# Leaving out the filler products on the tensor engine at both ends of an attention, MLP and soft-mixture kernel

## The reference, cut to what matters

```
# 1. chunked attention, B=4, H=8, S=768, D=64; chunks of 32 queries,
#    keys: 8 memory rows + 16 before the chunk + the chunk + 8 after it
a = softmax(q_c @ k_full.T / 8);  out[:, :, chunk] = a @ v_full
x = out as 3072 tokens x 512
# 2. MLP, 512 -> 2048 -> 512
h = x @ w_in;  g = h * sigmoid(h);  x = g @ w_out
# 3. soft mixture, 8 experts x 4 slots, 512 -> 1024 -> 512
logits = x @ phi                          # 3072 x 32
slot_input = softmax(logits, over tokens).T @ x
slot_out[e] = relu(slot_input[e] @ w1[e]) @ w2[e]
out = softmax(logits, over slots) @ slot_out
```

## Time and profile before

| | |
|---|---|
| median of 3 runs | 479.77 us (477.81 to 480.75) |
| the profiled execution's own time | 477.67 us |
| its span | 475.9 us |
| PE busy | 451.3 us, 95% of the span, 5460 passes |
| PE weight loads busy | 332.9 us, 70% |
| DVE, ACT, POOL busy | 275.0, 138.6, 45.3 us |
| DMA | 81.59 MB; share of the 16 engines 44.4% on average |
| chain that ended last | PE 85%, DMA 6%, DVE 4%, others 1% or less each |

### The profile page before, as it was taken

How to read it: one execution, slowest core, us unless ns; L and a number is a source line. 1 busy time by engine, 2 the same in 40 slices (tenths; PEclk the granted TensorE clock), 3 DMA queues, 4 the chain that set the end, 5 groups by cost and what they waited for, 6 DMA issues and landing times.

```text
span 475.9 us, 12278 instructions
## 1 busy us (share of the span) xinstructions
PE 451.3 (95%) x5460; PEld 332.9 (70%) x5460; DVE 275.0 (58%) x531; ACT 138.6 (29%) x255; POOL 45.3 (10%) x43
## 2 busy tenths in 40 slices
PE   5899999999999999999999999999999999899970
PEld 5799667777776787768777677777677878534540
DVE  5657458665596556766666676558444656532232
ACT  2665233233331333322233223333122212201121
POOL 2475000000000000000000000000000000100000
PEclk9999999999999999999999999999999999999996
DMA  8989222220222022202231122020350599999998
GB/s 334 420 314 386 70 91 101 102 99 16 88 101 67 37 99 101 101 3 100 102 101 57 45 101 101 3 89 2 128 227 0 199 359 417 422 364 425 419 384 287
DMA packets 19748, 81.59 MB, mean 171 GB/s; under 512 B 1648, under 2 KB 7920, under 8 KB 14064
## 3 DMA queue, kind: packets, MB, share of 16 engines
q1 hardware_dynamic: 19696, 80.81, 44.4%
HBM read 74.51 MB, written 6.29 MB: 170 GB/s over the span
## 4 chain that ended last, share of the span: by engine, by line
PE 85%; DMA 6%; DVE 4%; ACT 1%; POOL 1%; issue 1%; DVEq 0%; SPq 0%; POOLq 0%
PE h_ps L273 54%; PE o_ps L255 6%; DMA unit<-w 5%; PE lpu_ps L289 5%; PE lpu_ps L309 4%; PE sx_ps L232 3%; PE pt_ps L241 2%; PE sx_ps L309 2%; PE h_ps L940 1%; PE sx_ps L878 1%; POOL sc L757 1%; PE lpu_ps L297 1%; PE h_ps L878 1%; DMA qk_sb<-qk 1%; PE o_ps L920 1%
## 5 line engine op out<-in xcount | busy, mean ns | idle before, releaser
L273 PE MATMUL h_ps<-x_odd,wh 128*128 128x512 f32 x384 | 126.9, 400 | 0.0
L478 DVE SCALAR_TENSOR_TENSOR gT<-gT,h_ps 128x512 f32<-128x512 f32 (+1 forms) x108 | 66.5, 616 | 98.0 <-ACT gT L377 97.4
L377 ACT ACTIVATE gT<-h_ps 128x512 f32<-128x512 f32 (+1 forms) x108 | 58.5, 542 | 185.4 <-PE h_ps L273 184.4
L273 PEld LDWEIGHTS h_ps<-x_odd,wh 128*128 128x128 f32 x384 | 72.1, 188 | 21.3 <-issue 5.1
L273 PE MATMUL h_ps<-x_even,wh 128*128 128x512 f32 x256 | 85.0, 401 | 0.0
L273 PE MATMUL h_ps<-x_odd,wl 128*128 128x512 f32 x192 | 74.9, 390 | 0.0
L488 DVE STREAM_TRANSPOSE gB<-gT 128x512 f32<-128x512 f32 x80 | 56.7, 709 | 2.0
L273 PEld LDWEIGHTS h_ps<-x_even,wh 128*128 128x128 f32 x256 | 48.1, 188 | 12.5 <-issue 2.2
L757 POOL TENSOR_TENSOR sc<-sc,row_stats 128x512 f32<-128x512 f32 x24 | 25.1, 1044 | 280.4 <-DVE row_stats L462 280.4
L273 PE MATMUL h_ps<-x_short,wh 128*128 128x256 f32 x256 | 50.6, 290 | 0.3 <-DVE x_short L467 0.3
L273 PE MATMUL h_ps<-x_even,wl 128*128 128x512 f32 x128 | 49.9, 390 | 0.0
(11 more groups left out here) (167 smaller groups left out, 491.7 us busy)
## 6 DMA issues: line engine op xcount, KB each, us to landing
unit<-w SPq DMA_DIRECT2D x32, 1024.0 KB, 10.2
qk_sb<-qk SPq DMA_DIRECT2D x24, 640.0 KB, 4.2
v_sb<-v SPq DMA_DIRECT2D x24, 512.0 KB, 5.5
w_stage<-w_in SPq DMA_DIRECT2D x4, 1024.0 KB, 11.1
wot<-w_outT SPq DMA_DIRECT2D x4, 1024.0 KB, 11.3
unit<-w_out SPq DMA_DIRECT2D x4, 1024.0 KB, 6.2
out<-unit SPq DMA_DIRECT2D x4, 1024.0 KB, 8.4
out<-unit SPq DMA_DIRECT2D x2, 512.0 KB, 7.1
```

The source lines that it names most:

```text
L273: last = nc.tensor.matmul(h_ps[k % 2][:, 0:TOKS[b]], w[:, n, kc, q * 128:(q + 1) * 128], x[:, lo, kc, 0:TOKS[b]], start=(kc == 0 and w is ...
L377: nc.scalar.activation(gt_of(b, k), h_ps[k % 2][:, 0:TOKS[b]], ACT.Tanh, scale=0.5).then_inc(tanh_done, 1)
L478: nc.vector.scalar_tensor_tensor(out=gt_of(b, k), in0=gt_of(b, k), scalar=1.0, in1=h_ps[k % 2][:, 0:TOKS[b]], op0=ALU.add, op1=ALU.mult).t ...
```

## The change

All calls of `keep_busy` are left out, and the function with them. No other instruction is changed, added or moved, on any engine.

```diff
             pe.wait_ge(const_set, 5)
-            keep_busy(2, h_ps[0])
             pe_scores(pe, 0)
-            keep_busy(2, h_ps[0])
             pe_scores(pe, 1)
-            keep_busy(10, h_ps[0])
             pe_probs_T(pe, 0)
-            keep_busy(4, h_ps[0])
             pe_values(pe, 0)
             pe_probs_T(pe, 1)
             pe_scores(pe, 2)
             pe_values(pe, 1)
-            keep_busy(4, h_ps[0])
             for b in range(NB):
                 pe_block(pe, b)
             pe.wait_ge(acc_done, 4 * LAST)
-            keep_busy(6, s_ps)
             pe_logits(pe, LAST, NF - 1)
-            keep_busy(3, s_ps)
             pe_fold(pe, LAST)
-            keep_busy(9, s_ps)
             pe_dispatch(pe, LAST, NUN)
...
             last.then_inc(uf_mm, 1)
-            keep_busy(3, h_ps[0])
             pe.wait_ge(uf_cp, 1)
...
             last.then_inc(uT_tr, 1)
-            keep_busy(3, h_ps[0])
             pe.wait_ge(uT_done, 1)
...
             last.then_inc(si_mm, 1)
-            keep_busy(3, h_ps[0])
             pe.wait_ge(si_cp, 1)
...
-            keep_busy(3, h_ps[0])
             pe.wait_ge(siT_done, 1)
...
-            keep_busy(3, ex_ps)
             slot_outputs(pe, 1)
-            keep_busy(4, ex_ps)
             for i in range(ROUNDS):
                 outputs(pe, 1, i)
```

More of the change, by code:

```diff
@@ L875, in _ @@
         def _(pe):
-            def keep_busy(count, idle_ps):
-                for _ in range(count):
-                    nc.tensor.matmul(idle_ps[:, 0:128], fold[:], ident[:], start=True, stop=True)
             pe.wait_ge(const_set, 5)
-            keep_busy(2, h_ps[0])
             pe_scores(pe, 0)
-            keep_busy(2, h_ps[0])
             pe_scores(pe, 1)
-            keep_busy(10, h_ps[0])
             pe_probs_T(pe, 0)
-            keep_busy(4, h_ps[0])
             pe_values(pe, 0)
```

## The result

The changed kernel is slower by 0.56%: 482.0 us median of 20 runs (479.94 to 482.76) against 478.66 of 20 runs of the kernel before; ratio 1.0056, 95% interval [1.0044, 1.0068], about 2.7 us, which is also the difference of the two means; the medians are 3.3 us apart. The forecast was +1.65 us on 479.77, and 481.4.

A forecast was written before the change was run, and what follows sets the result against it. Only the two ends, chains through PE, were taken to matter; PE bounds what lies between 19 and 403 us. +0.85 - 0.45 + 1.7 - 0.45 = +1.65 us on 479.77 gave 481.4 us, range 478.1 to 485.4.

The forecast's parts named there:

- The faster rival: Whole kernel: the clock costs nothing, fillers only stood in line; -1.3 us, 478.5 us; chance 0.10.
- no fall: Last end: the 2.8 us gap brings no fall of the clock; first end +0.85, tail -0.9, 479.7 us; chance 0.24.
- slow through the tail: Last end: clock stays low to the product with w_out, +7 in place of +1.7, 486.7 us; chance 0.08.
- Late rise: First end: only the MLP lifts the clock, second values and first MLP steps slow; +3.0, 483.6 us; chance 0.16.
- First end: Start to 19 us: earlier work -0.4, low clock +1.25, together +0.85 (-0.4 to +3); first MLP step at 19.8 us.
- the +0.75 for the values: First end: the first values, 32 passes, slow at the low clock, 1.9 us; part of the clock's +1.25.
- I expect the rise while the third scores or the second values run: First end: gapless work from the values on lifts the clock there; +2.0 for the clock if second values are slow too.
- To the product with w_out: Last end from 403 us: no fillers in the way -0.45; clock falls at about 408 us (two in three), +1.7.
- the forecast's +1.7 for the dispatch: Last end: the clock falls at about 408 us, so the last dispatch runs slow, in 4 us; +1.7.
- The transfers follow: Last end: each us the product with w_out moves shifts the four loads at 419.58 us and all behind them.
- Outputs, forecast -0.45: Last end, second `slot_outputs` and outputs: without their 14 filler passes 0.45 us earlier, the clock taken as held.
- a gap of that size is borne; I take the clock as held: Last end: PE's 1.79 us wait for the last load brings no fall of the clock, so outputs gain 0.45 us.

## Why the prediction was right, and where its terms were not

*Direction and mechanism.* Right: the fillers' own time is worth little, the clock is worth more. The faster rival fell with the transposition at 11.3 us at 1.12; "no fall" and "slow through the tail" fell with the two profiles of the changed kernel, which both show a fall at 408 to 409 and the product with w_out at the upper level again (3.64 us in both, as before). "Late rise" in its full form (into the first MLP steps) was seen in no profile.

*First end, forecast +0.85.* The fillers' own share was about right (second scores at 6.40 for 6.3, DVE 0.25 us earlier for 0.33), and so were the slow transposition (1.12, forecast 1.22) and values (1.98, forecast 1.90). No row or run shows the +0.75 for the values that the sum uses; it was the author's estimate, and the runs showed +0.83. What failed is the step "I expect the rise while the third scores or the second values run". It is true of two profiles (19.91 and 20.02 us, one of them the kernel with only this end changed) and not of the first (20.84). Forecast was 19.8. The base was off as well: 18.98 came of an early rise, and the six profiles with all first fillers average 19.26. The three without any average 20.26, so the difference is 1.0 us, near the +1.1 that the runs give for this end alone. That the forecast of +0.85 is close to this is in part luck: it missed both the slow values and the late base, and the two errors offset each other.

*To the product with w_out, forecast -0.45 + 1.7.* Measured in the profiles +1.4: the end of the last MLP step to the dispatch 5.68 us for 6.00 (-0.3; the fold takes 0.70 for 0.60, which I had not counted), the dispatch to its end 4.08 for 2.34 (+1.7). No row or run ahead of this one shows the forecast's +1.7 for the dispatch; it was the author's estimate, and it was right to a tenth.

*The transfers follow.* Right: +3.42 at the issue became +3.50 at the last landing.

*Outputs, forecast -0.45.* This is the step that failed: "a gap of that size is borne; I take the clock as held". Both profiles of the changed kernel have a fall there, and in the first the delay grows by 1.1 us between the last landing and the first store of the second half. Only 0.2 us of that stand ahead of the outputs (3.36 us after the last expert for 3.19), where the missing fillers give back most of what the clock costs; 0.9 is the slow first round. The reason given was a single execution in which the clock had held. The kernel before itself falls there in about half of its executions, in the second profile at +1.57, so the fillers around slot_outputs don't secure what they are there for; taking them out alone costs nothing that can be measured (0.9986).

*The size.* The two mis-sized terms add about 1 + 1.6 us in the profiles. But the profiled execution of the kernel before (477.67 us) lies 1.4 us below the mean of its 20 runs, and that of the changed kernel (482.15) 0.4 us above the mean of its own. Hence 4.5 us between two profiles and 2.7 between means. That the forecast time of 481.4 comes within 0.6 us of the measured median is luck as well: by the medians the change was put 1.7 us too low, and the base, a median of three runs, was 1.1 us too high (479.77 for 478.66). Four of the changed kernel's 20 times lie at 480.24 and below, apart from the other sixteen (481.45 and up). Their granted clocks are 0.984 to 0.989, those of the sixteen 0.977 to 0.981, and the profile's 0.979. A fall of 6.8 us less, as an estimate from that profile, would make it 0.986. So these four very likely had one fall less or shorter ones; which, no profile shows.

## What to carry to other kernels

Filler on the tensor engine paid here where it filled a wait behind which the clock was low without it, and ended before the wait did: with ten products at the first end the transposition took 0.66 us and not 1.12, with nine ahead of the last dispatch this took 2.3 us and not 4.1. Each did what all the groups of their end did; no run has these nineteen alone. Put it where PE is already idle, and look at the first real instruction after it, in more than one execution: at the lower level the same ten products took 4.36 us instead of 2.50 and outlasted their wait. Cutting groups on the chain by a product or two gave nothing that could be measured by itself. And profile the kernel before more than once: behind the same wait of 1.79 us for the last load the clock stayed at 1.00 in one execution and fell to 0.50 in another, and then both the base and the gain are means over two cases.

## What the runs showed of the hardware that I had not expected

The clock's changes were not tied to the instruction. With the same first end the rise came at 7.0, 7.1, 8.2, 8.5, 10.1 and 10.6 us, and in the changed kernel at 16.8 and 19.5, each estimated from the lengths of the rows around it; the span of the cost is 0.4 us at the first end of the kernel before (first MLP step at 18.98 to 19.41) and 0.9 in that of the changed one (19.91 to 20.84). The clock was lowered when PE was already busy again: in the second profile of the kernel before it fell at 460.6, 1.4 us into work that followed a wait of 1.79 us, and was low until 464.1 under unbroken fillers and products.
